# Linear attention with decay in a mixed kernel: the attention stage rewritten as 64x64 TensorE tiles on two half-chunks

## What is computed

```
for t in range(S):                                   # S = 768
    kt, vt, rt = (k[:, :, t], v[:, :, t], r[:, :, t])
    cur = einsum('bhd,bhe->bhde', u[None] * kt, vt)
    y[:, :, t] = einsum('bhd,bhde->bhe', rt, state + cur)
    state = w[None, :, :, None] * state + einsum('bhd,bhe->bhde', kt, vt)
x = y as [3072, 384]
logits = x @ phi; d = softmax over tokens; c = softmax over slots
slot_out[e] = relu((d.T @ x)[e] @ w1[e]) @ w2[e];  x = c @ slot_out
second MoE: expert of the largest x @ w_gate, h = relu(x_e @ w1[e]), y_e = h @ w2[e]
```

## Time and profile before

| | us |
|---|---|
| median of three runs | 339.49 |
| span of the profiled execution | 338.2 |
| PE busy | 314.9 (93%) |
| DVE busy | 213.1 (63%) |
| POOL busy | 98.9 (29%) |
| ACT busy | 88.5 (26%) |

### The profile page before, as it was taken

How to read it: one execution, slowest core, us unless ns; L and a number is a source line. 1 busy time by engine, 2 the same in 40 slices (tenths; PEclk the granted TensorE clock), 3 DMA queues, 4 the chain that set the end, 5 groups by cost and what they waited for, 6 DMA issues and landing times.

```text
span 338.2 us, 7016 instructions
## 1 busy us (share of the span) xinstructions
PE 314.9 (93%) x2589; PEld 269.1 (80%) x2589; DVE 213.1 (63%) x363; ACT 88.5 (26%) x156; POOL 98.9 (29%) x91
## 2 busy tenths in 40 slices
PE   7889979899988999698999999899999999999993
PEld 7678867788877878587763349699999999999992
DVE  7898868999889898789553402583534353342512
ACT  0333224224223242223221012352222222222210
POOL 7565454673647465547320000000000000000000
PEclk9999989999999999999999999989999999999997
DMA  5967987899899999995898932700200102020202
GB/s 98 222 154 195 270 191 243 191 289 221 250 247 210 289 184 315 297 212 158 280 370 339 418 156 63 311 0 2 94 0 35 58 0 93 0 93 0 93 3 98
DMA packets 13750, 56.99 MB, mean 169 GB/s; under 512 B 1984, under 2 KB 5152, under 8 KB 11936
## 3 DMA queue, kind: packets, MB, share of 16 engines
q1 hardware_dynamic: 12720, 45.68, 49.6%
q10 hardware_dynamic: 1008, 11.01, 8.8%
HBM read 51.97 MB, written 4.72 MB: 168 GB/s over the span
## 4 chain that ended last, share of the span: by engine, by line
PE 47%; DMA 2%; issue 2%; POOL 1%; DVE 1%; SPq 1%; ACT 0%; DVEq 0%; POOLq 0%
PE ps L1146 10%; PE ps L1145 10%; PE ps L1147 10%; PE ps L1130 4%; PE ps L1017 3%; PE ps L1040 3%; DMA wraw<-wb 2%; PE ps L884 1%; PE ps L995 1%; PE ps L1049 1%; PE ps L1027 1%; PE ps L949 1%; PE ps L956 1%; PE ps L923 1%; DVE acc L842 1%
## 5 line engine op out<-in xcount | busy, mean ns | idle before, releaser
L831 DVE SCALAR_TENSOR_TENSOR hl<-ps,hh 128x512 fp32r<-128x512 f32 x48 | 32.9, 689 | 59.0 <-ACT hh L566 59.0
L1145 PE MATMUL ps<-w2h,hh 128*128 128x384 f32 x192 | 64.6, 337 | 0.0
L1146 PE MATMUL ps<-w2l,hh 128*128 128x384 f32 x192 | 64.5, 336 | 0.0
L1147 PE MATMUL ps<-w2h,hl 128*128 128x384 f32 x192 | 64.2, 334 | 0.0
L923 PE MATMUL ps<-rp,kb 112*128 112x128 f32 x384 | 50.3, 285 | 12.0 <-DVE kb L647 11.2
L923 PEld LDWEIGHTS ps<-rp,kb 112*128 112x128 f32 x384 | 45.7, 195 | 17.2 <-issue 12.0
L566 ACT ACTIVATE hh<-ps 128x512 fp32r<-128x512 f32 x48 | 28.6, 600 | 76.0 <-PE ps L1130 76.0
L436 POOL TENSOR_TENSOR dl<-rk,dh 112x512 fp32r<-112x512 f32 x24 | 31.4, 1307 | 38.1 <-ACT dh L477 38.1
L426 POOL TENSOR_TENSOR rk<-ind 112x512 f32<-112x512 f32 x24 | 33.8, 1408 | 26.8 <-DMA intk<-tmaj 24.7
L661 DVE TENSOR_TENSOR pt<-ps,mask 128x512 f32<-128x512 f32 x48 | 33.0, 690 | 9.3 <-PE ps L923 8.4
L1146 PEld LDWEIGHTS ps<-w2l,hh 128*128 128x128 f32 x192 | 36.1, 188 | 1.6
(11 more groups left out here) (173 smaller groups left out, 385.9 us busy)
## 6 DMA issues: line engine op xcount, KB each, us to landing
ind<-dmaj SPq DMA_DIRECT2D x48, 288.0 KB, 5.6
wearly<-wa ACTq DMA_DIRECT2D x7, 1536.0 KB, 9.0
intk<-tmaj SPq DMA_DIRECT2D x24, 384.0 KB, 6.7
wearly<-wa SPq DMA_DIRECT2D x4, 1536.0 KB, 10.0
out<-acc SPq DMA_DIRECT2D x5, 768.0 KB, 3.5
wlate<-wa SPq DMA_DIRECT2D x4, 768.0 KB, 4.4
wlate<-wa SPq DMA_DIRECT2D x2, 1536.0 KB, 8.8
wmid<-wa SPq DMA_DIRECT2D x1, 1536.0 KB, 6.4
```

The costliest lines, as they stand in the source:

```text
L831: v.scalar_tensor_tensor(out=hl[:, f % 4, :], in0=ps[:, f % 4, :], scalar=0.0, in1=hh[:, f % 4, :].bitcast(F32), op0=ALU.max, op1=ALU.subt ...
L1145: mm(o, a_h, w2h[:, f, :], start=(f == 0), stop=False)
L1146: mm(o, a_h, w2l[:, f, :], start=False, stop=False)
L1147: ins = mm(o, a_l, w2h[:, f, :], start=False, stop=(f == KF - 1))
```

## The change

It rewrites the attention stage. Attention's 24 steps are chunk-major now (`c, ip = divmod(n, PAIRS)`) and all written out, so the code of every engine is longer. Each 128-token chunk is treated as two halves of 64 tokens (`HALF`): scores are only made within a half, and the state advances twice a step, from `sta` (into the chunk) to `stb` (into its second half) and on to the next `sta`. Every pair keeps its own state. Matmuls of scores, increments, carried state and masked scores use quarter tiles of the array, 64 rows by 64 columns, with row tile and column tile alternating over head, half and batch, and each row tile with its own bank. `ind` holds r and k alone, in four slots; v's dimension-major copy is not loaded. The two scalings are one DVE instruction (`pre`, L575, 1024 columns, two steps ahead). The u term is 16 matmuls with one moving column (u) a step, L834, whose sums DVE copies onto the diagonal of the masked scores with one predicated copy (L612). ACT, not DVE, takes the output out of its bank (`xs`, L456). `wusb` and the first two steps are loaded without a wait; PE waits for the small weights before step 0. Lines below are those of the changed kernel.

```diff
@@ sync @@
-                    sp.wait_ge(y_done, n + 1 + 1)
-                    sp.wait_ge(dv_done, n + 1 + 1)
-                    load(c % 3, n + 3)
+            for n in range(4, STEPS):
+                sp.wait_ge(pre_ready, n - 3)
+                sp.wait_ge(rk_ready, n - 3)
+                load_d(n)
+                sp.wait_ge(y_done, n - 3)
+                load_t(n)
@@ vector @@
+            def pre(n):
+                dve.wait_ge(ind_in[n % 4], (n // 4 + 1) * 32)
+                wait(dve, y_done, n - 2)
+                tab_ = tab[0:R2, n % PAIRS, :, :].unsqueeze(2).to_broadcast([R2, 2, 2 * B, HALF])
+                v.tensor_tensor(rkb[0:R2, n % 3, :, :].rearrange("p i (g t) -> p i g t", t=HALF),
+                                ind[0:R2, n % 4, :, :].rearrange("p i (g t) -> p i g t", t=HALF), tab_,
+                                ALU.mult).then_inc(pre_ready, 1)
...
+                dve.wait_ge(sc_done, n + 1)
+                v.tensor_tensor(pt[:, :, :, :], ps[:, SC:SC + 2, 0:B * HALF].rearrange("p j (b t) -> p j b t", b=B),
+                                causal, ALU.mult).then_inc(pt_ready, 1)
+                dve.wait_ge(inc_done, n + 1)
+                update(stb[0:R2, ip, :, :], sta[0:R2, c % 2, ip, :, :], 0, True)
+                dve.wait_ge(pt_ready, n + 1)
+                v.copy_predicated(pt[:, :, :, :], on_diag,
+                                  ps[:, SC:SC + 2, B * HALF:B * HALF + B].unsqueeze(3).to_broadcast([P, 2, B, HALF])
+                                  ).then_inc(att_ready, 1)
+                if c < NC - 1:
+                    dve.wait_ge(st_ready, sub_a(n))
+                    update(sta[0:R2, 1 - c % 2, ip, :, :], stb[0:R2, ip, :, :], 1, False)
+                if n + 2 < STEPS:
+                    pre(n + 2)
@@ tensor @@
-                mm(ps[0:R2, DB, :], onesr[0:R2, :], dl[0:R2, :], start=False, stop=True).then_inc(d_done, 1)
...
+            def scores(n):
...
+                            mm(ps[toks[m], SC + j, B * HALF + b:B * HALF + b + 1],
+                               rk[rows[j], n % 2, b * C + m * HALF:b * C + (m + 1) * HALF],
+                               wusb[rows[j], 1, n % PAIRS:n % PAIRS + 1], start=True, stop=True,
+                               skip_group_check=True)
...
+                            ins = mm(ps[toks[m], SC + j, b * HALF:(b + 1) * HALF], rkb[rows[j], n % 3, 1, at_],
+                                     rkb[rows[j], n % 3, 0, at_], start=True, stop=True, skip_group_check=True)
...
+            for n in range(STEPS):
+                if n == 0:
+                    scores(n)
+                    increments(n)
+                else:
+                    increments(n)
+                    scores(n)
+                pe.wait_ge(st_ready, sub_a(n))
+                wait(pe, xs_ready, n)
+                carried(n, True)
+                if n:
+                    turn(n - 1)
+                    logits(n - 1)
+                pe.wait_ge(in_done, n + 1)
+                carried(n, False)
+                within(n)
```

More of the change, by code:

```diff
@@ L185, in mixed_kernel @@
         small_in = sem("small_in")
[L186 removed]
+        ind_in = [sem(f"ind_in{i}") for i in range(4)]
+        tok_in = [sem(f"tok_in{i}") for i in range(4)]
         dch = sem("dch")
@@ L391, in _ @@
             g = nc.gpsimd
-            for s, start in starts["pool"].items():
-                pool.sem_inc(s, start)
             n = [0]
@@ new lines, in _ @@
+            v.tensor_tensor(wk[0:R2, :, 0, :], tab[0:R2, :, 1, :], half, ALU.mult)
+            v.tensor_tensor(wk[0:R2, :, 1, :], tab[0:R2, :, 1, :], half, ALU.mult).then_inc(wk_ready, 1)
+            dve.wait_ge(wk_ready, 1)
+            link(scale_tables(0, 1))
+            pre(0)
+            link(scale_tables(1, PAIRS))
+            pre(1)
+            dve.wait_ge(consts, NCONST)
+            for rows in (slice(0, HB), slice(HB, P)):
+                v.tensor_copy(mask[rows, :], strict[rows, rows])
+                last_ins = v.tensor_copy(diag[rows, :], ident[rows, rows])
@@ L952, in pe_step @@
-                for b in range(B):
-                    if b % 2 == 0:
-                        pe.wait_ge(att_ready, n * 2 + b // 2 + 1 + 1)
-                    for j in range(2):
-                        ins = mm(ps[j * HB:j * HB + D, YB, b * C:(b + 1) * C],
-                                 intk[:, k3, 1, b, j * D:(j + 1) * D], pt[:, k2, b, j, :],
-                                 start=(c == 0 and b == 0), stop=(b == B - 1), skip_group_check=True)
-                ins.then_inc(y_done, 1)
-            with pe.Fori(0, PAIRS - 1) as ip:
-                for c in range(NC):
-                    pe_step(ip, c)
@@ new lines, in carried @@
+            def carried(n, swap):
+                c, ip = divmod(n, PAIRS)
+                for b in range(B):
+                    for j in range(2):
+                        m = 1 - j if swap else j
+                        st = stb[rows[j], ip, b, :] if m else sta[rows[j], c % 2, ip, b, :]
+                        ins = mm(ps[rows[j ^ b % 2], YB + m, b * HALF:(b + 1) * HALF], st,
+                                 rkb[rows[j], n % 3, 0, b * C + m * HALF:b * C + (m + 1) * HALF],
+                                 start=(swap and b < 2), stop=False, skip_group_check=True)
+                if swap:
+                    ins.then_inc(in_done, 1)
@@ new lines, in within @@
+            def within(n):
+                pe.wait_ge(att_ready, n + 1)
+                for b in range(B):
+                    for m in range(2):
+                        for j in range(2):
+                            ins = mm(ps[rows[j ^ b % 2], YB + m, b * HALF:(b + 1) * HALF],
+                                     intk[toks[m], n % 4, 1, b, j * D:(j + 1) * D], pt[toks[m], j, b, :],
+                                     start=False, stop=(b >= 2), skip_group_check=True)
+                ins.then_inc(y_done, 1)
@@ new lines, in turn, with logits @@
+            def turn(n):
+                wait(pe, tok_done, n)
+                for b in range(B):
+                    ins = nc.tensor.transpose(ps[:, TB, b * P:b * P + R2], xs[0:R2, b, :], ident[0:R2, 0:R2])
+                ins.then_inc(t_done, 1)
+            def logits(n):
+                c, ip = divmod(n, PAIRS)
+                if ip == 0:
+                    wait(pe, lts_ready, c)
+                for b in range(B):
+                    ins = mm(ps[b * NS:(b + 1) * NS, LB, c % 4 * P:c % 4 * P + P], phisb[0:R2, b % 2, ip, :],
+                             xs[0:R2, b, :], start=(ip == 0), stop=(ip == PAIRS - 1), skip_group_check=True,
+                             tile_position=(0, b * NS))
+                ins.then_inc(lg_done, 1)
```

468 lines of the change are left out of this document (174 added, 294 removed).

## The result

The changed kernel takes 356.78 us (median of 4, 354.73 to 362.71), the kernel before, timed beside it, 339.12 (4 runs). The ratio is 1.0489, 95% interval 1.041 to 1.0569: slower, where the prediction said faster by a tenth and put 336 at the top of its range.

The account below looks back on a forecast made before the run. PE, DVE and loads stood near each other; loads gave 6.0 of 6.38 us a step. New steps at 5.0: 13.5 + 23 x 5.0 + 3.5 = 132.0 against 166.6, so 303.6, plus 1.3: 305 us, range 291 to 336.

Parts of the forecast that it names:

- The tiles run four wide: TensorE in attention: four 64x64 tiles run side by side, 0.0135 us a record, 2.04 us a step; two-by-two rival 13%.
- The loads: Attention's DMA: 0.786 MB a step, 3.74 us, or 5.03 us while weight pieces flow.
- DVE and the predicated copy: DVE in attention: mask 0.69, updates 0.41 each, `pre` 1.53, predicated copy 0.69; 3.95 us a step, at the top 4.8.
- The first mask: Start of attention: PE waits for the small weights until 11.0; scores and signal done about 13.5 us.
- The end: From last mask to copy of the last output 3.5 us, then the unchanged 171.6 us.
- The step: Each attention step: chain 4.65 us, loads 5.03 for most steps, taken as 5.0; TensorE's own work 3.02.
- a clock below 0.9: Sign in the changed trace: granted clock below 0.9 in attention would make the prediction fall.
- The clock rival: TensorE in attention: clock stays low, chain 7.5 us a step, 364 us; half the time low, 331 us; chance 10%.

Follow-up runs that it names:

- all_fill3: Changed kernel with TensorE's chunks from 1 through the last as one loop and three full-tile matmuls a step before the carried state: 322.04 us, ratio 0.9461.
- b_idle: Kernel before with three unread 512-column memsets on DVE in each step, so that TensorE stands idle before its scores: 376.1 us.
- turnfirst: Changed kernel with transposes and logits of the step before moved ahead of the first carried-state matmuls: 353.0 us.
- loop_fillq: `loop_fill4` with twelve quarter-tile matmuls in place of the four full-tile ones: 389.65 us (one run).
- statefirst: Changed kernel with DVE's first state update moved ahead of the mask: 351.1 us.
- fill4: Changed kernel, still unrolled, with four unread 128x128 matmuls between scores and carried state of steps 1 to 23: 365.8 us.
- fill4q: `fill4` with each weight piece cut into four DMAs of 384 KB: 360.3 us.
- sf_fill3q: Changed kernel with DVE's state update first, weight pieces cut in four, and three full-tile matmuls before the carried state: 359.6 us.
- nou: Changed kernel without the u term's one-column matmuls after the first step, so its output lacks the u term: 328.5 us.
- loop_fill4: `loop` with four full-tile 128x128 matmuls between scores and carried state: 331.7 us; timed again, 334.38 us, ratio 0.9824.
- all_fill2: `loop_fill4` with the last chunk in the loop too and two full-tile matmuls in place of four: 323.74 us, ratio 0.9545.
- loop: Changed kernel in a loopable form, with TensorE's chunks 1 to 4 (16 of 24 steps) as one loop: 360.3 us.

## Why the prediction was wrong, point by point

- *The tiles run four wide*: right. 0.026 us a record at 0.50 and 0.0144 (by group 0.012 to 0.016) at 1.00, where the sum had 0.0135 (2.04 us a step). The Trainium skill's rule ("TensorE: Matmul & The Clock Gate", section "Wait — 56ns, not 53.3ns?"), no start-to-start below about 25 ns, does not hold across four tiles here: the page's number is met by accident, at half clock.
- *The loads*: right in size. 0.786 MB a step; the DMA share was 0.62 and no wait for loads was longer than one of 4.4 us at the start. They bounded nothing; in `all_fill3` 4.9 us a step on average were sustained with the pieces, at a share of 0.86, so the 5.03 us was slightly too much.
- *DVE and the predicated copy*: right. 0.72 us against 0.69, the update 0.41, `pre` 1.55 against 1.53, TensorE's wait for `stb` 1.3 us a step against 1.5.
- *The first mask*: 17.2 us instead of 13.5, and in a place that was not looked at: DVE is as good as never idle from 3.2 us on (0.2 us before the memset), and behind the two `pre` stand four copies of mask and diagonal and a memset, 5.4 us, which the sum left out. The path through TensorE, which the sum had, was over by 13.9. This is 3.7 us of the miss.
- *The end*: 353.4 - 177.4 = 176.0 us from the last mask, where 3.5 + 171.6 = 175.1 were foretold. 0.9 us.
- *The step*: the rest, 23 x (6.97 - 5.00) = 45.2 us, and this is the step that failed: the sum took all of TensorE's terms, 3.02 us a step, at the higher clock. They ran at a mean granted clock of 0.57, and TensorE was busy for 130 us instead of 72; the prediction had named a clock below 0.9 as a sign of its fall. The argument that failed is its own: "Against: in shorter idle times before, attention kept a mean of 0.99". That row told of 128-wide work. The clock rival was worked out (7.5 us a step, 364 us with the level always low; measured 7.17 as the median step, 357) and given 10%, of which the range took in the milder half. It was priced as a matter of idle time; `b_idle`, `turnfirst` and `loop_fillq` show that it is a matter of which tiles the work is in. That quarter tiles were named in the same sentence, with nothing in the trace of before to weigh them by, should have widened the range past 336.
- *Not in the sum at all*: the instruction fetch. The diff turns a loop into 24 copies of 344 records. At the half clock this cost little (standstills of 3.7 us in all), but it takes the gain away as soon as anything is mended: standstills of 17 to 33 us in the six unrolled kernels that had a shorter chain or a higher clock (`turnfirst`, `statefirst`, `fill4`, `fill4q`, `sf_fill3q`, `nou`). The Trainium skill ("Runtime: NRT & Kernel Launch", section "Instruction fetch mechanics") says that blocks of 256 instructions are fetched ahead and the cost is mostly hidden. The size agrees with the 16 KB and some 250 records a packet here. That it is hidden holds in the kernel before, where TensorE has no such standstill and the packets of its first MoE come 10 to 17 us apart, and not for records of 0.012 to 0.026 us.

With both mended, the forecast's mechanism is there: on average 4.9 us a step in the loop of `all_fill3` against 5.0 foretold, 322 us in all. That the two agree so closely is in part luck, since three fillers and the jumps are in the one and 5.03 us of loads bounded the other. What lies between 322 and 305 is mainly the slow start: the first eight steps of `all_fill3` take 59.6 us, 21 more than at the 4.8 of the loop, with a clock of 0.69. The three fastest kernels beat the kernel before by 4.5 to 6%, and the changed one with it.

What stays open: why the clock is granted to one mixture of tiles and not to another. Without fillers, and with twelve in quarter tiles, it wasn't held; with three or four full ones no timed execution of the looped kernels came near the 354 us of the lower level; with two, one of five did. How the slow start splits into fetch and clock is open too. Whether the 48-row and one-column matmuls count for less than a filled 64x64 tile was not tried apart from `nou`.

## What to carry to other kernels

Splitting TensorE's array bought time here only where the clock stayed up: look for granted clock first in any kernel whose main work moves from full to small tiles, and try a few full-tile matmuls in the waits. Count records too: when a record shrinks to 0.012 to 0.016 us, as here at the higher clock, straight code can be fetched slower than it runs, so try a loop whose body is a few steps (a jump cost 0.4 us). And if mending one bound changes nothing, mend it together with the next one before calling it harmless.

## What the runs showed of the hardware

- Matmuls in four 64x64 tiles side by side, with 32-bit operands and at most 64 moving columns, take 0.012 to 0.016 us a record at the higher clock (`all_fill3`) and 0.019 to 0.026 at the lower (changed kernel).
- TensorE was granted 0.50 for 100 us on end while busy 99.8% of the time, with quarter tiles (`loop_fillq`); the same kernel with four full-tile matmuls in place of twelve quarter-tile ones had 1.00 (`loop_fill4`).
- One and the same kernel (`all_fill2`) took 322 us (mean clock 0.92) or 354 us (0.78, with 0.50 in its loop).
- Instruction packets (16 KB, some 250 records of TensorE) came 3.4 to 5.8 us apart in the changed kernel's attention, 5.9 to 8.2 beside a weight piece, and a TensorE that stood without instructions went on 1.2 to 1.75 us after one had landed. A loop body of four steps, some 1,400 records, was fetched once (`loop`: no packet from 71 to 155 us).
- Each turn of that loop cost about 0.4 us at the jump (`all_fill3`, 5.17 against 4.78 us).
